# Three-stage kernel on one core: down products respread, the first phase's last step moved inside pair 0, weights scaled while split

## What is computed

```python
state = gamma * state + k_t v_t^T ; y_t = scale * q_t state     # 4 x 8 heads, 768 steps, 64 wide
h = x @ w_in ; g = where(h >= 1, h, where(h <= -1, 0, (h + 1)**2 / 4)) ; x = g @ w_out   # 3072 x 512, d_ff 2048
h = x @ w_in ; e = exp(h - max(h)) ; solu = h * e / (sum(e) + 1e-9)                      # d_ff 1024
ln = (solu - mean) / sqrt(var + 1e-6) * g_ln ; out = ln @ w_out
```

## Time and profile before

| what | value |
|---|---|
| time, median of 3 runs | 886.77 us (886.26 to 888.0) |
| profiled execution, its own time | 886.03 us |
| its span, first to last instruction | 884.2 us |
| TensorE busy | 862.4 us (98%), mean granted clock 0.994 |
| VectorE, ScalarE, GpSimd busy | 448.3 (51%), 332.1 (38%), 244.2 (28%) |

### The profile page before, as it was taken

One profiled execution on the slowest core, in us unless ns is written; L12 is line 12 of the kernel. 1 busy time (PEld: TensorE's weight loads), 2 busy tenths in 40 slices (PEclk: granted clock), 3 DMA queues, 4 the chain that ended last, 5 costly groups with the idle time before them and its releaser, 6 DMA issues.

```text
span 884.2 us, 12102 instructions
## 1 busy us (share of the span) xinstructions
PE 862.4 (98%) x4816; PEld 702.3 (79%) x4816; DVE 448.3 (51%) x772; ACT 332.1 (38%) x505; POOL 244.2 (28%) x234
## 2 busy tenths in 40 slices
PE   8999999999999999999999999999889999999898
PEld 7788878888888888888888788877767888888686
DVE  5555443334333243233433333677698878888820
ACT  2433342213221132122312232345466765566531
POOL 2644532232223222322211212238212311111000
PEclk9999999999999999999999999999999999999999
DMA  9921111111111202111111003210444455555341
GB/s 342 355 78 49 48 49 49 48 60 38 60 48 48 75 10 96 48 49 37 48 48 36 24 1 143 95 48 18 138 156 131 151 187 164 155 153 167 108 143 47
DMA packets 50744, 82.85 MB, mean 94 GB/s; under 512 B 5248, under 2 KB 23680, under 8 KB 50688
## 3 DMA queue, kind: packets, MB, share of 16 engines
q1 hardware_dynamic: 50688, 82.08, 28.6%
HBM read 56.90 MB, written 25.17 MB: 93 GB/s over the span
## 4 chain that ended last, share of the span: by engine, by line
PE 88%; DVE 5%; ACT 2%; issue 2%; DMA 1%; SPq 1%; POOL 0%; DVEq 0%
PE acc L413 29%; PE h L383 28%; PE o_ps L940 14%; PE p L883 9%; PE att L320 2%; PE att L331 2%; PE att L355 1%; PE att L345 1%; DVE solu L1111 1%; DMA q<-in_q 1%; DVE zT_lo L1143 1%; DVE h L1057 1%; ACT solu L985 0%; PE acc L331 0%; DVE zq L1134 0%
## 5 line engine op out<-in xcount | busy, mean ns | idle before, releaser
L413 PE MATMUL acc<-g_hi,w 128*128 128x512 f32 x768 | 258.5, 398 | 2.6 <-POOL g_lo L734 2.6
L383 PE MATMUL h<-x_hi,w 128*128 128x512 f32 x760 | 250.0, 390 | 2.4 <-DVE g_raw L668 1.9
L734 POOL TENSOR_TENSOR g_lo<-g_raw,g_hi 128x512 fp32r<-128x512 f32 x96 | 124.9, 1301 | 394.4 <-ACT g_hi L458 394.4
L508 ACT ACTIVATE g_raw<-g_raw,half_bias 128x512 f32<-128x512 f32 x96 | 69.5, 724 | 334.4 <-DVE g_raw L663 334.4
L413 PEld LDWEIGHTS acc<-g_hi,w 128*128 128x128 f32 x768 | 144.9, 189 | 38.4 <-issue 3.4
L383 PEld LDWEIGHTS h<-x_hi,w 128*128 128x128 f32 x760 | 142.7, 188 | 32.9 <-DVE g_raw L668 2.3
L663 DVE TENSOR_SCALAR g_raw<-h 128x512 f32<-128x512 f32 x96 | 66.2, 690 | 167.8 <-PE acc L413 167.7
L413 PE MATMUL acc<-g_lo,w 128*128 128x512 f32 x384 | 150.3, 392 | 0.0
L383 PE MATMUL h<-x_lo,w 128*128 128x512 f32 x380 | 147.9, 389 | 0.0
L668 DVE TENSOR_TENSOR g_raw<-h,g_raw 128x512 f32<-128x512 f32 x96 | 66.4, 692 | 70.1 <-ACT g_raw L508 70.1
L458 ACT ACTIVATE g_hi<-g_raw 128x512 fp32r<-128x512 f32 x96 | 60.7, 632 | 73.7 <-DVE g_raw L668 73.7
(11 more groups left out here) (116 smaller groups left out, 1063.8 us busy)
## 6 DMA issues: line engine op xcount, KB each, us to landing
z<-zq SPq DMA_DIRECT2D x24, 512.0 KB, 2.8
zt<-z SPq DMA_DIRECT2D x96, 128.0 KB, 3.1
kT<-in_kT SPq DMA_DIRECT2D x24, 256.0 KB, 2.8
q<-in_q SPq DMA_DIRECT2D x24, 256.0 KB, 2.6
v<-in_v SPq DMA_DIRECT2D x24, 256.0 KB, 2.9
x2T<-y SPq DMA_DIRECT2D x24, 256.0 KB, 2.5
x_raw<-x2T SPq DMA_DIRECT2D x12, 512.0 KB, 4.2
out<-o SPq DMA_DIRECT2D x24, 256.0 KB, 4.3
```

Of the source, the lines that this page charges most:

```text
L383: last = mm(hb[f % 2][:, :], ww, xx[:, kt, :], start=kt == 0 and t == 0, stop=kt == KT - 1 and t == 2)
L413: last = mm(acc[m][:, :], ww, gg[:, f % 2, :], start=f == 0 and t == 0, stop=f == FT1 - 1 and t == 2)
L508: nc.scalar.activation(gate[:, f % 2, :], gate[:, f % 2, :], ACT.Square, bias=half_bias[:, 0:1], scale=0.5).then_inc(sem["squared"], 1)
L734: tt(g[1][:, f % 2, :], gate[:, f % 2, :], g[0][:, f % 2, :].bitcast(F32), ALU.subtract)\
```

## The change

On TensorE the last step's `up(15)` goes between products 7 and 4 of pair 0, its three downs stay behind `up(0)`; a table DOWNS says which downs follow which up. On VectorE `join` is cut in parts (`join_p2` to `join_p3`, one for each product, their instructions unchanged); `clamp(15)` stands between the parts for products 7 and 4 of pair 0, `larger(15)` before that for product 5; in pair 1 `split_z(0)` stands between the parts; the join of pair 11 is spread into the chain of pair 10. On ScalarE the last step's square and high part stand ahead of the first exponential, and the outputs follow DOWNS. The output weights are scaled by ScalarE's split and by VectorE's low part (8 of each), not by 8 instructions of their own; GpSimd's 8 low parts go to VectorE, and the two low parts of pair 1's x go from VectorE to GpSimd. VectorE's low parts of the weights move one step later, so that the high part was made a step before. Stores on SyncE's queue follow DOWNS.

```diff
@@ -445,12 +445,8 @@
...
-            def last_step():
-                up(BLOCKS - 1, FT1 - 1)
-                for f in range(FT1 - LAG - 1, FT1):
-                    down(BLOCKS - 1, f)
-
-            finish["pe_last_step"] = last_step
+            finish["pe_up"] = lambda: up(BLOCKS - 1, FT1 - 1)
+            finish["pe_down"] = lambda f: down(BLOCKS - 1, f)
 
         @block.scalar
         def _(act):
@@ -491,10 +487,12 @@
...
-                for piece in {10: (0,), 12: (1, 2, 3), 13: (4,), 14: (5, 6, 7)}.get(f, ()):
-                    act.wait_ge(sem["w2_scaled"], piece + 1)
-                    copy(mem["w2_out"][0][:, piece, :], mem["w2_out_raw"][:, piece, :])\
-                        .then_inc(sem["w2_out_hi"], 1)
+                if f == 10:
+                    act.wait_ge(sem["gains"], 16)
+                for piece in {10: (0, 1), 11: (2,), 12: (3, 4, 5, 6), 13: (7,)}.get(f, ()):
+                    act.wait_ge(sem["w2_out_loaded"][piece], 16)
+                    nc.scalar.activation(mem["w2_out"][0][:, piece, :], mem["w2_out_raw"][:, piece, :], ACT.Copy,
+                                         scale=mem["g_ln"][:, piece:piece + 1]).then_inc(sem["w2_out_hi"], 1)
...
@@ -629,32 +627,30 @@
...
                         .then_inc(sem["w2_summed"], 1)
-                if f == 6:
+                if f == 7:
                     dve.wait_ge(sem["w2_summed"], 4)
-                for kt in {6: (0,), 7: (1,), 8: (2, 3)}.get(f, ()):
...
                     dve.wait_ge(sem["w2_in_hi"], kt + 1)
                     tt(mem["w2_in"][1][:, kt, :], raw[:, kt, :], mem["w2_in"][0][:, kt, :].bitcast(F32),
...
+                for i in {10: (0, 1), 11: (2,)}.get(f, ()):
                     dve.wait_ge(sem["w2_in_hi"], KT + i + 1)
                     tt(mem["w2_sum"][1][:, i, :, :], sums[:, i, :, :], mem["w2_sum"][0][:, i, :, :].bitcast(F32),
                        ALU.subtract).then_inc(sem["w2_in_lo"], 1)
-                if f == 9:
+                if f == 11:
                     dve.wait_ge(sem["gains"], 16)
-                for piece in {9: (0, 1), 10: (2, 3, 4), 11: (5, 6, 7)}.get(f, ()):
-                    dve.wait_ge(sem["w2_out_loaded"][piece], 16)
-                    nc.vector.tensor_scalar(mem["w2_out_raw"][:, piece, :], mem["w2_out_raw"][:, piece, :],
-                                            mem["g_ln"][:, piece:piece + 1], None, ALU.mult)\
-                        .then_inc(sem["w2_scaled"], 1)
-                if f in (12, 14):
-                    n = (f - 12) // 2
-                    dve.wait_ge(sem["x2_hi"], 2 * n + 1)
-                    dve.wait_ge(sem["x2_summed"], 4 * n + 4)
-                    tt(mem[f"x2_{n}"][1][:, :, :], mem[f"x2_{n}_raw"][:, :, :],
-                       mem[f"x2_{n}"][0][:, :, :].bitcast(F32), ALU.subtract).then_inc(sem["x2_lo"], 1)
-                    dve.wait_ge(sem["x2_hi"], 2 * n + 2)
-                    tt(mem[f"x2_sum{n}"][1][:, :, :, :], mem[f"x2_sum{n}_raw"][:, :, :, :],
-                       mem[f"x2_sum{n}"][0][:, :, :, :].bitcast(F32), ALU.subtract).then_inc(sem["x2_lo"], 1)
+                for piece in {11: (0, 1), 12: (2,), 13: (3, 4, 5), 14: (6, 7)}.get(f, ()):
+                    dve.wait_ge(sem["w2_out_hi"], piece + 1)
+                    nc.vector.scalar_tensor_tensor(
+                        mem["w2_out"][1][:, piece, :], mem["w2_out_raw"][:, piece, :],
+                        mem["g_ln"][:, piece:piece + 1], mem["w2_out"][0][:, piece, :].bitcast(F32),
+                        ALU.mult, ALU.subtract).then_inc(sem["w2_out_lo"], 1)
+                if f == 12:
+                    for i, name in enumerate(("x2_0", "x2_sum0")):
+                        dve.wait_ge(sem["x2_hi"], i + 1)
+                        dve.wait_ge(sem["x2_summed"], 4)
+                        tt(mem[name][1][:], mem[f"{name}_raw"][:], mem[name][0][:].bitcast(F32), ALU.subtract)\
+                            .then_inc(sem["x2_lo"], 1)
 
             def clamp(blk, f):
                 n = blk * FT1 + f
@@ -745,13 +741,6 @@
...
-                        for piece in {13: (0, 1), 14: (2, 3)}.get(f, ()):
-                            w2_out_lo(piece)
-
-            def w2_out_lo(piece):
-                pool.wait_ge(sem["w2_out_hi"], piece + 1)
-                tt(mem["w2_out"][1][:, piece, :], mem["w2_out_raw"][:, piece, :],
-                   mem["w2_out"][0][:, piece, :].bitcast(F32), ALU.subtract).then_inc(sem["w2_out_lo"], 1)
 
             def sums_of_x2(n):
 
@@ -769,7 +758,14 @@
...
-            finish["pool_w2_out"], finish["pool_sums"] = w2_out_lo, sums_of_x2
+            def second_x2_lo():
+
+                for i, name in enumerate(("x2_1", "x2_sum1")):
+                    pool.wait_ge(sem["x2_hi"], 3 + i)
+                    tt(mem[name][1][:], mem[f"{name}_raw"][:], mem[name][0][:].bitcast(F32), ALU.subtract)\
+                        .then_inc(sem["x2_lo"], 1)
+
+            finish["pool_x2_lo"], finish["pool_sums"] = second_x2_lo, sums_of_x2
             finish["pool_low"] = lambda: low(BLOCKS - 1, FT1 - 1)
 
             nc.gpsimd.memset(mem["power"][:, :], -0.5).then_inc(sem["power_set"], 1)
@@ -798,6 +794,10 @@
...
+
+    DOWNS = {1: (0,), 2: (1, 2), 3: (3, 4), 4: (5,), 5: (6, 7), 6: (8, 9), 7: (10,), 8: (11, 12), 9: (13, 14),
+             10: (15,)}
+    FIRST_LEFT = 16
...
@@ -851,24 +851,24 @@
...
-                if n >= 4:
-                    store(2 * n - 7)
-                if n >= 3:
-                    store(2 * n - 6)
+                for s in DOWNS.get(n - 1, ()):
+                    store(s)
                 put_z(2 * n)
                 put_z(2 * n + 1)
                 get_z(2 * n)
                 get_z(2 * n + 1)
                 if n == 0:
                     finish["store_x2"]()
-            for s in range(TILES - 9, TILES - 6):
-                store(s)
+            store(15)
+            store(16)
             put_z(TILES - 2)
+            store(17)
             put_z(TILES - 1)
+            store(18)
             get_z(TILES - 2)
-            store(TILES - 6)
+            store(19)
             get_z(TILES - 1)
-            for s in range(TILES - 5, TILES):
+            for s in range(TILES - 4, TILES):
                 store(s)
             for par in range(2):
                 sp.wait_ge(sem["o_stored"][par], 16 * (TILES // 2))
@@ -905,12 +905,13 @@
...
-                pe.wait_ge(sem["x2_lo"], 2 * n + 2)
+                pe.wait_ge(sem["x2_lo"], 2 * n + 1)
                 product(bank_of(n, 1), a(0, FIRST), b(0, LEFT))
                 wait(pe, sem["h_max"], 2 * n)
                 product(bank_of(n, 2), a(1, FIRST), b(1, LEFT))
                 if n == 0:
                     pe.wait_ge(sem["gmax"], BLOCKS * FT1 - 1)
+                pe.wait_ge(sem["x2_lo"], 2 * n + 2)
                 product(bank_of(n, 6), s(1), t(1))
                 if n == 0:
                     pe.wait_ge(sem["part_copied"], 1)
@@ -918,6 +919,7 @@
...
                 if n == 0:
+                    finish["pe_up"]()
                     pe.wait_ge(sem["taken"], 1)
...
@@ -944,12 +946,11 @@
...
                 if n == 0:
-                    finish["pe_last_step"]()
-                if 3 <= n < PAIRS2 - 2:
-                    down(2 * n - 5)
-                if 2 <= n < PAIRS2 - 2:
-                    down(2 * n - 4)
-            for s in range(TILES - 9, TILES):
+                    for f in range(FT1 - LAG - 1, FT1):
+                        finish["pe_down"](f)
+                for s in DOWNS.get(n, ()):
+                    down(s)
+            for s in range(FIRST_LEFT, TILES):
                 down(s)
 
         @block.scalar
@@ -967,6 +968,7 @@
...
                 wait(act, sem["h_max"], 2 * n)
+                wait(act, sem["sq_sum"], 2 * n)
                 copy(part, bank_of(n, 1)[:, :]).then_inc(sem["part_copied"], 1)
 
...
@@ -1004,16 +1006,16 @@
...
             copy_part(0)
+            finish["act_square"]()
+            finish["act_high"]()
             exponential(0, SECOND)
             exponential(0, FIRST)
             squares(0, SECOND)
-            finish["act_square"]()
-            finish["act_high"]()
+            squares(0, FIRST)
             normalize(0, SECOND)
-            squares(0, FIRST)
             normalize(0, FIRST)
             finish["act_evacuate"]()
-            for n in range(1, PAIRS2 - 1):
+            for n in range(1, PAIRS2 - 2):
                 copy_part(n)
                 split_x(n + 1)
                 split_z(2 * n - 2)
@@ -1024,30 +1026,40 @@
...
                 normalize(n, SECOND)
                 normalize(n, FIRST)
-                if 3 <= n < PAIRS2 - 2:
-                    output(2 * n - 5)
-                if 2 <= n < PAIRS2 - 2:
-                    output(2 * n - 4)
-            n = PAIRS2 - 1
+                for s in DOWNS[n]:
+                    output(s)
+            n = PAIRS2 - 2
             copy_part(n)
+            split_x(n + 1)
+            split_z(2 * n - 2)
```

(120 more changed lines are left out.)

8 lines of the change are left out of this document (4 added, 4 removed).

## The result

| | before | after |
|---|---|---|
| median | 887.01 us (4 runs) | 872.88 us (4 runs, 871.96 to 873.97) |
| ratio, 95% interval | | 0.984 (0.9823 to 0.9858) |
| profiled execution: its time, span, last matmul's start | 886.03, 884.2, 880.70 | 873.97, 872.2, 868.67 |

What follows compares the result with a forecast made beforehand. TensorE is busy 98% of the span, with VectorE pacing early pairs. 603.0 + 255.7 of matmuls + 8.8 of stalls + six slow first matmuls at 0.1 = 868.1, 12.8 less: profiled 873.2, median 874.0 us, range 869.5 to 878.5.

Steps and rivals of the forecast that it cites:

- E: The end of step 14 of the last block on TensorE, forecast at 603.0 us.
- (a): At down(15): TensorE waits for GpSimd's low(15), a stall of 1.65 us; before it was 2.74 and the clock.
- (b): In up(1): product 4 of pair 1 waits for the evacuated banks, a new stall of 2.3 us.
- (c): At down(0): TensorE waits for the first low half after pair 0's second turn, a new stall of 1.95 us.
- (d): Product 3 of pair 2 waits for the first join on VectorE, stall 0.7 us; before it was 4.38 and the clock.
- (e): At down(2): TensorE waits for its z, a stall of 0.4 us.
- c: The start of clamp(15) on VectorE, inside pair 0, forecast at 619.85 us.
- Rival 2: VectorE's and GpSimd's turns don't bite and pair 0's chain is 2 us shorter: 870 us, chance 0.08.
- Rival 3: All TensorE gaps go, 22.2 us less: 864.6 us, chance 0.03.
- rival 4: More lost in front: every turn lost (1.5 more), clock falling twice (2 to 3, not covered): 877.8 us, chance 0.13.
- Rivals 5 and 6: 5: output(17) holds tile 20 or down(19), 878 us, chance 0.07; 6: VectorE's chain bounds the middle, 888.5, 0.04.
- Rival 7: Waits only moved: pair 0's softmax, 7 us later, goes straight through to the end: 886.5 us, chance 0.03.

Runs made afterwards that it cites:

- the repeat: The changed kernel run once more with nothing altered, beside the kernel before: 873.12 us, ratio 0.9856 (0.9837 to 0.9875).

## Why the prediction held, step by step

| step of the prediction | forecast | profile after |
|---|---|---|
| gap before `up(13)` | gone | gone |
| E | 603.0 | 604.13 |
| product 6 of pair 0 | 1.8 | 1.26 |
| (a) `down(15)` | 1.65 | 1.79 |
| (b) product 4 of pair 1 | 2.3 | 2.57 |
| clock behind (b) | left out | 1.6 |
| (c) `down(0)` | 1.95 | 0.09 |
| (d) product 3 of pair 2 | 0.7 | 0.31 |
| (e) `down(2)` | 0.4 | 0.62 |
| slow first matmuls, rest | 0.6 | 0.8 |
| sum of losses behind E | 9.4 | 9.1 |
| last matmul ended by the pace | 868.1 | 868.90 |

**The replay.** Adding durations of before in the new order placed every gap, named who ends it, and missed none. The evacuation was put at c + 14.75 and ended at 634.55 + 1.25 = c + 15.0 (c = 620.80); the first join of pair 2 was put at c + 34.35 and stands at 655.16, c + 34.36. The idle time ahead of the last `clamp` was put at 9 and is 8.90. GpSimd's x parts ran from 610.50 to 615.3, forecast 610 to 615, and nobody waited for them; the middle and the last eight downs lost nothing, as forecast. Taking back parts gives the sizes: 1.9 for the preparation, 6.5 for `down(0)` between ups 1 and 2, 5.4 to 5.7 for the end. What the last step's move does is negative, 4.5. Together they are 9.3 to 9.6 of the 12.7 us by which the repeat is faster. The rest, over 3 us, no run took back by itself; the gap of 1.36 before product 3 of pair 3, which is gone, and the slow matmuls behind the old wait of 2.74 are the likely places.

**Clock: forecast wrong, effect right.** The prediction said that the clock would not fall, since its longest idle time was 2.15 against the 2.58 of before; it fell after 2.41 in the profiled execution. A fall by the waits of pair 1 was one of the prediction's own signs of being wrong, so on this point it was wrong: 2.58 was the shortest wait in one profile behind which the clock fell, and no bound. It also said what a fall would do: it would be covered but for about 1 us by the waits behind it. That is seen. The slow matmuls lost 1.6, and `down(0)`, whose z comes when it comes, lost 0.09 and not 1.95. In the kernel with x on VectorE the gap was 2.51 and the clock stayed full: there `down(0)` lost 1.91. So (c) was right, and the time it stands for went into the slow matmuls instead. The sum was kept right by this cover, which the prediction had named, and not by luck. Nor does the clock fall in every execution. One fall takes 0.002 off the mean clock, as in the repeat's profile (0.998). Of the four executions of the changed kernel two have 0.996 and two 1.0, which leaves no room for a fall; these two took 872.14 and 871.96 us, and the fastest of the repeat, at 0.998, took 872.02. That also speaks for a covered fall.

**Product 6.** The turns are real, but were dosed 0.5 too high: `clamp(14)` starts 1.8 behind E and not 2.4. Three pieces at step 13 took 3.59 beside GpSimd's sums and its low part; one alone takes 0.74.

**E.** Forecast 603.0, from the kernel before; the profiled execution lost more in its first 20 us. The first 20 us of the changed kernel, then those of the kernel with both end edits taken back, whose first phase is the same:

```profile
0.00:20.00 20.00, 16.98 (x159) 14.39 (x160) 8.96 (x15) 5.32 (x9) 3.78 (x9) 0.91 0.93 332
```

```profile
0.00:20.00 20.00, 18.30 (x172) 15.64 (x173) 10.75 (x17) 5.93 (x10) 4.92 (x9) 1.00 0.94 337
```

Here 159 matmuls ran in that time, there 172; from 20 to 600 us TensorE is then busy for 579.50 us in both. The last matmul of product 2 starts at 606.62 here, and at 605.96, 605.84, 605.49, 605.17, 605.08 and 604.23 in the six other profiled executions with the same code up to there. So E varies by 2.4 from execution to execution, 603.0 lies inside (601.7 to 604.1), and the difference is no effect of the change. The wait of 1.6 for q and the clock of 0.91 explain a part of it only: the repeat had neither and still reached 605.84. It fits that the profiled execution of after is 1.1 above its median: the forecast of 873.2 for the profiled one was 0.8 low, and that for the median, which added 0.74, was 1.1 high. Both lie within the scatter of the four runs (871.96 to 873.97), so that they came this close is in part luck.

**The end.** The prediction credited the vanished gap to the spread join, "4 us early". The runs show that `down(15)` between the ups does it by itself; the mechanism named was sufficient, not necessary. Its "slack 0.7" for a whole join behind one down holds at pair 11: no gap.

**What it never asked.** The steps (a) to (c) with the clock cost 6.05 us and were summed as the price of a good edit. The prediction had the sentence that decides it, that VectorE waits for 9 us with the softmax of pair 0 queued behind it, and priced the waits that follow. It did not price the order of before with the other edits in place: there `down(15)` waits 0.9 more, product 6 and `down(2)` lose what they lose now, and (b), (c) and (d) are gone. The sum for the change was right; which part brought it was not in it.

**Rivals.** Rival 2 (no turns) falls with the 8.65 against 4.44 us. Rival 3 (all gaps go) falls with the 9.1 that are left, rival 4 (more lost in front) with product 6, which lost 1.26 and not more than 1.8, and with the one fall of the clock, which was covered. Rivals 5 and 6 find no gap behind 664. Rival 7 was half true: pair 0's softmax is late by some 9 us (join 4 at 621.41 instead of 611.08, 1.5 of it from the executions' starts), and 4.5 of that reach the end.

## What to carry to other kernels

An instruction of an in-order engine that waits long is paid by all that is queued behind it, so put it where the work behind it has no reader yet, and price each part of a bundled edit against leaving it where it was. Work moved to GpSimd to relieve VectorE isn't free for VectorE: where VectorE's instruction takes two tensors from SBUF in the same microseconds, add the durations; the joins, which take one of their two from PSUM, kept theirs (0.68 us). When two edits cure one gap, each may cure it alone; take the simpler one.

## What was not expected of the hardware

**Turns between VectorE and GpSimd.** Five VectorE instructions of 128x512 took 8.65 us beside three GpSimd ones and 4.44 beside one; a single one took 2.27 instead of 0.74. GpSimd's x parts grew from 2.40 to 2.84 at the same time: the loser waits until the other's instruction has ended, and GpSimd's are the long ones.

**The clock near 2.5 us of idle time.** Losses at one gap, from start to start, and whether the clock fell to its lower level: in the profiled executions it fell after 2.57, 2.60, 2.61, 2.62, 2.73, 2.74 and all longer ones (3.59 to 4.38), and it didn't after 1.91, 2.06, 2.48, 2.51 and, in one kernel, 2.73. Two kernels with the same gap of 2.73 at the same instruction went either way, and the one that had a further gap of 1.24 some 18 us earlier kept its clock. Whether that is the kernel or the single execution isn't settled: in the changed kernel itself, behind the gap of 2.57 to 2.61, two executions of four have no room for a fall in their mean clock. From 1.4 to 2.5 us are lost in slow matmuls each time.
